# Attention in front of two MoE layers: how the softmax reciprocals reach the output rows, and a new order of the evictions

## What is computed

```python
q_rot, k_rot = rotate(q), rotate(k)                     # rotary embedding over D
scores = np.matmul(q_rot, k_rot.transpose(0, 1, 3, 2)) / np.sqrt(D)
attn = np.exp(scores - scores.max(-1, keepdims=True))
attn = attn / (attn.sum(-1, keepdims=True) + 1e-9)
x = np.matmul(attn, v)                                  # then heads side by side: 2304 x 512
gate, val = sigmoid(x @ w_gate), x @ w_val              # 512 -> 1536
x = (gate * val) @ w_out                                # 1536 -> 512
h = x @ w_in                                            # 512 -> 1024
ln = layernorm(h * softmax(h)) * g_ln
return ln @ w_out2                                      # 1024 -> 512
```

## Time and profile before

| | |
|---|---|
| median of the runs | 960.77 us (960.64 to 960.99) |
| profiled execution | 960.94 us, span 959.1 us |
| TensorE busy | 948.4 us (99%) |
| DVE busy | 508.2 us (53%) |
| ACT busy | 363.5 us (38%) |
| POOL busy | 339.1 us (35%) |
| attention | about the first 290 us of the span |

### The profile page before, as it was taken

One profiled execution on the slowest core, in us unless ns is written; L12 is line 12 of the kernel. 1 busy time (PEld: TensorE's weight loads), 2 busy tenths in 40 slices (PEclk: granted clock), 3 DMA queues, 4 the chain that ended last, 5 costly groups with the idle time before them and its releaser, 6 DMA issues.

```text
span 959.1 us, 15452 instructions
## 1 busy us (share of the span) xinstructions
PE 948.4 (99%) x5442; PEld 793.8 (83%) x5442; DVE 508.2 (53%) x890; ACT 363.5 (38%) x783; POOL 339.1 (35%) x246
## 2 busy tenths in 40 slices
PE   8999999999999999999999999999999999999998
PEld 6888888888876889888888888888888888888886
DVE  6898988989973343323234233243444554444441
ACT  5787787877862111111111111111111343333332
POOL 5556465564402904103202302401756432222200
PEclk9999999999999999999999999999999999999999
DMA  3333332333220120200100100100120011111111
GB/s 111 96 89 87 88 89 78 90 86 88 61 92 1 67 66 1 66 1 1 66 0 1 67 1 1 44 0 0 44 87 0 1 23 23 22 22 22 22 22 44
DMA packets 31842, 42.34 MB, mean 44 GB/s; under 512 B 5696, under 2 KB 20288, under 8 KB 31808
## 3 DMA queue, kind: packets, MB, share of 16 engines
q1 hardware_dynamic: 31664, 41.73, 15.6%
q10 hardware_dynamic: 144, 0.15, 0.1%
HBM read 28.30 MB, written 4.72 MB: 34 GB/s over the span
## 4 chain that ended last, share of the span: by engine, by line
PE 94%; ACT 1%; DVE 1%; issue 1%; POOL 1%; DMA 1%; SPq 0%; POOLq 0%; DVEq 0%
PE ps L1125 31%; PE ps L1169 15%; PE ps L1232 10%; PE ps L1062 9%; PE ps L1207 9%; PE ps L1107 8%; PE ps L1089 8%; PE ps L1029 2%; PE ps L1217 2%; PE ps L1000 1%; DMA raw_w<-in_moe_w_out 1%; DVE nmax L862 0%; ACT prob L702 0%; POOL x_lo L665 0%; POOL w_lo L554 0%
## 5 line engine op out<-in xcount | busy, mean ns | idle before, releaser
L1125 PE MATMUL ps<-x_hi,w_hi 128*128 128x512 f32 (+1 forms) x480 | 177.1, 369 | 0.2 <-POOL w_lo L554 0.2
L1125 PE MATMUL ps<-x_lo,w_hi 128*128 128x512 f32 (+1 forms) x480 | 176.7, 368 | 0.0
L1125 PE MATMUL ps<-x_hi,w_lo 128*128 128x512 f32 (+1 forms) x480 | 176.6, 368 | 0.0
L929 DVE TENSOR_TENSOR hid<-ps,sig 128x512 f32<-128x512 f32 (+1 forms) x60 | 38.3, 638 | 234.3 <-PE ps L1125 206.4
L741 ACT ACTIVATE sig<-ps 128x512 f32<-128x512 f32 (+1 forms) x60 | 33.3, 555 | 295.5 <-PE ps L1125 295.5
L1062 PE MATMUL ps<-kT,qT 128*128 128x288 f32 (+2 forms) x672 | 121.9, 309 | 2.3 <-ACT prob L702 1.9
L862 DVE TENSOR_REDUCE nmax<-ps 128x1 f32<-128x576 f32 x144 | 108.6, 755 | 23.3 <-PE ps L1062 19.4
L604 POOL TENSOR_SCALAR w_hi<-raw_w 128x1024 fp32r<-128x1024 f32 x15 | 41.3, 2778 | 210.5 <-PE ps L1169 210.5
L702 ACT ACTIVATE prob<-ps,nmax 128x576 f32<-128x576 f32 x128 | 94.2, 740 | 47.0 <-DVE nmax L862 45.7
L1125 PEld LDWEIGHTS ps<-x_hi,w_hi 128*128 128x128 f32 x480 | 90.5, 189 | 16.1 <-issue 0.9
L1125 PEld LDWEIGHTS ps<-x_hi,w_lo 128*128 128x128 f32 x480 | 90.5, 189 | 15.0
(11 more groups left out here) (120 smaller groups left out, 1659.2 us busy)
## 6 DMA issues: line engine op xcount, KB each, us to landing
kT<-kT SPq DMA_DIRECT2D x30, 288.0 KB, 3.7
raw_k<-in_k SPq DMA_DIRECT2D x16, 288.0 KB, 2.8
raw_q<-in_q SPq DMA_DIRECT2D x16, 288.0 KB, 3.1
out_y<-y_sb SPq DMA_DIRECT2D x36, 128.0 KB, 2.3
v_sb<-in_v SPq DMA_DIRECT2D x64, 64.0 KB, 2.3
raw_w<-in_moe_w_gate SPq DMA_DIRECT2D x6, 512.0 KB, 3.7
raw_w<-in_moe_w_val SPq DMA_DIRECT2D x6, 512.0 KB, 4.7
raw_w<-in_moe_w_out SPq DMA_DIRECT2D x6, 512.0 KB, 5.6
```

What stands on the lines that cost most here:

```text
L929: nc.vector.tensor_tensor(hid[:, f, 0:n], gv_ps[f][1][:, 0:n], sig[:, f, 0:n], ALU.mult).then_inc(hid_ready, 1)
L1125: last = nc.tensor.matmul(in_parts(gv_ps[f][n][:, 0:size(c)], c), w, x, start=m == 0, stop=m == len(todo) - 1)
```

## The change

1. INV writes its nine reciprocals to a block of 128 columns that is zero elsewhere. One transpose (RT) turns them, ACT copies nine rows of 128 to `rinv_t`, SP writes these to a DRAM tensor `inverses` (RW), waits, and reads them back to `rrep` by two DMAs whose source names each head's row 64 times (RR). `rwide`, R and KTR's third block are gone; KTR is now KT. `normal` waits for these DMAs (`rrep_in`). A slot order (`place`) puts the four rows of a head side by side.
2. kT and kTs hold the second head's last 64 keys a second time (one more piece of T), so that S8's products of the second head are two of 288 columns per part and no longer of 288, 224 and 64.
3. Evictions: ACT has A3, B1, TQ, B0, A0, B2, A1 and KT; DVE has A2, K and B3. Before, ACT had A0, B2, TQ, B0, A3, KTR and R, DVE A2, K, A1, B3 and B1.
4. New orders on all engines, SP's among them; POOL's RQ works one pair further ahead and XL one step earlier. SP issues the first weights in step 15 ahead of that step's RW.

```diff
-            kTT.append(alloc(at, f"kT{u}", [P, 4 * S + 2 * TAIL], F32R))
-            kT.append(kTT[u][:, 0:2 * S])
-            kTs.append(kTT[u][:, 2 * S:4 * S])
+            kTT.append(alloc(at, f"kT{u}", [P, 4 * S + 3 * TAIL], F32R))
+            kT.append(kTT[u][:, 0:2 * S + TAIL])
+            kTs.append(kTT[u][:, 2 * S + TAIL:4 * S + 2 * TAIL])
...
-        rinv = alloc(at, "rinv", [P, 2, SLOTS])
-        rwide = alloc(at, "rwide", [P, SLOTS, D])
+        rinv = alloc(at, "rinv", [P, 2, P])
+        rinv_t = alloc(at, "rinv_t", [SLOTS, P])
...
-        ORDER_PE = ["A2", "A0", "S0", "K", "B2", "S1", "A1", "B3", "S2", "TQ", "k", "S3", "T", "PV0", "KTR", "S4",
-                    "R", "q", "B1", "S5", "B0", "S6", "PV1", "S7", "A3", "S8"]
-
-        ORDER_ACT = ["A0", "S0", "B2", "S1", "TQ", "k", "T", "S2", "S3", "KTR", "R", "S4", "q", "B0", "S5", "S6",
-                     "S7", "A3", "S8"]
-
-        ORDER_DVE = ["A2", "S0", "K", "S1", "A1", "B3", "S2", "INV", "S3", "k", "T", "S4", "PV0", "S5", "S6", "q",
-                     "B1", "S7", "PV1", "S8"]
-
-        ORDER_POOL = ["RQ", "XL", "RK"]
-        FIRST_PE = ["S0", "S1", "S2", "k", "S3", "T", "S4", "S5", "q", "B1", "S6", "B0", "S7", "A3", "S8"]
-        FIRST_ACT = ["S0", "S1", "S2", "k", "S3", "T", "S4", "S5", "q", "S6", "B0", "S7", "A3", "S8"]
-        FIRST_DVE = ["S0", "S1", "S2", "S3", "k", "S4", "T", "S5", "S6", "q", "B1", "S7", "S8"]
-        AHEAD = {"A0": -1, "A1": -1, "A2": -1, "B2": -1, "B3": -1, "K": -1, "TQ": -1, "KTR": -1, "R": -1,
-                 "PV0": -1, "PV1": -1, "INV": -1, "XL": -2, "k": 1, "q": 1, "T": 1, "RQ": 1, "RK": 2}
+        ORDER_PE = ["A2", "S0", "A3", "K", "S1", "RT", "B1", "B3", "k", "S2", "KT", "T", "S3", "PV0", "S4", "TQ",
+                    "B0", "q", "S5", "A0", "S6", "PV1", "S7", "B2", "S8", "A1"]
+        ORDER_ACT = ["A3", "S0", "RT", "B1", "S1", "k", "S2", "T", "KT", "S3", "TQ", "S4", "B0", "q", "S5", "A0",
+                     "S6", "B2", "S7", "A1", "S8"]
+        ORDER_DVE = ["A2", "S0", "INV", "K", "S1", "B3", "S2", "S3", "k", "T", "S4", "PV0", "S5", "S6", "q", "S7",
+                     "PV1", "S8"]
+        ORDER_POOL = ["RK", "RQ", "XL"]
+        ORDER_SP = ["RW", "RR", "LK", "T", "LQ", "LV"]
+        FIRST_PE = ["S0", "S1", "S2", "k", "S3", "T", "S4", "B0", "S5", "q", "A0", "S6", "B2", "S7", "A1", "S8"]
+        FIRST_ACT = ["S0", "S1", "S2", "k", "S3", "T", "S4", "B0", "S5", "q", "A0", "S6", "B2", "S7", "A1", "S8"]
+        FIRST_DVE = ["S0", "S1", "S2", "S3", "k", "S4", "T", "S5", "S6", "q", "S7", "S8"]
+        AHEAD = {"A2": -1, "A3": -1, "B1": -1, "B3": -1, "K": -1, "TQ": -1, "KT": -1, "RT": -1, "PV0": -1, "PV1": -1,
+                 "INV": -1, "XL": -1, "k": 1, "q": 1, "T": 1, "RQ": 2, "RK": 2, "RW": -1, "RR": -1, "LK": 2, "LQ": 2,
+                 "LV": 1}
...
-                return [(around, q_tail, odd), (tails, k_tail, odd)]
+                again = keys[u][:, 2 * S:2 * S + TAIL]
+                return [(around, q_tail, odd), (tails, k_tail, odd), (again, k_tail[:, 1, :], odd)]
...
+        inverses = nc.dram_tensor("inverses", (SLOTS, P), F32, kind="Internal").ap()
+        def place(j):
+            return j % 2 * MT + j // 2 if j < 2 * MT else j
...
+            def write_inverses(p, step):
+                bank, before = use("RT", step)
+                sp.wait_ge(tr_out[bank], before + 1)
+                sp.dma_start(inverses, rinv_t[:]).then_inc(inverses_out, 16)
+            def spread_inverses(p):
+                sp.wait_ge(inverses_out, num(p) * 16 + 16)
+                main = inverses[0:2 * MT, :].rearrange("(h t) n -> h (t n)", h=2)
+                tails = inverses[2 * MT:SLOTS, :].rearrange("o (h n) -> (o h) n", h=2)
+                for src, a, b in ((main, 0, MAIN), (tails, MAIN, S)):
+                    sp.dma_start(rrep[:, a:b], src.unsqueeze(1).broadcast_to([2, D, b - a])).then_inc(rrep_in, 16)
             def step_in(name, p, step):
-                if name == "RK":
+                if step == PAIRS - 1 and name == "RW":
+                    for bank, before in newest(PIECES, PAIRS - 1):
+                        sp.wait_ge(tr_full[bank], before + 1)
+                    weights(0)
+                if name == "LK":
                     load(p, k, raw_k, k_in, k_prod)
-                elif name == "QN":
+                elif name == "LQ":
                     load(p, q, raw_q, q_in, q_prod)
                 elif name == "T":
                     swap(p, step)
-                elif name == "VN":
+                elif name == "LV":
                     load_v(p)
-
-            AHEAD.update(QN=2, VN=1)
+                elif name == "RW":
+                    write_inverses(p, step)
+                elif name == "RR":
+                    spread_inverses(p)
...
-                    held = ("K", "AB"[j % 2] + str(j // 2)) if j < 2 * MT else ("TQ", "KTR")
+                    held = ("K", "AB"[j % 2] + str(j // 2)) if j < 2 * MT else ("TQ", "KT")
...
-                                     accum_out=rsum[:, par(p), j, 0:1]).then_inc(exp_done, 1)
+                                     accum_out=rsum[:, par(p), place(j), 0:1]).then_inc(exp_done, 1)
...
-                if name in ("R", "KTR") and not early(p, 1):
-                    act.wait_ge(x_norm[1], num(p))
-                if name == "R":
-                    nc.scalar.activation(rrep[:, 0:MAIN], src, ACT.Copy).then_inc(tr_out[bank], 1)
+                if name == "RT":
+                    if not early(p, 1):
+                        act.wait_ge(x_norm[1], num(p))
+                    nc.scalar.activation(rinv_t[:], src[0:SLOTS, 0:P], ACT.Copy).then_inc(tr_out[bank], 1)
                     return
-                if name == "KTR":
-                    for h in range(2):
-                        r0 = h * TAIL
-                        nc.scalar.activation(rrep[r0:r0 + TAIL, MAIN:S],
-                                             src[r0:r0 + TAIL, 2 * P + r0:2 * P + r0 + TAIL], ACT.Copy)
                 for dst, part in p_parts(name, src, par(p)):
                     last = nc.scalar.activation(dst, part, ACT.Copy)
...
-                    bank, before = use("R", at_pair(p, -1 - AHEAD["R"]))
+                    bank, before = use("RT", at_pair(p, -1 - AHEAD["RT"]))
                     dve.wait_ge(tr_full[bank], before + 1)
                 u = par(p)
                 nc.vector.tensor_reduce(rtot[:, u, :], rsum[:, u, :, :], AX.X, ALU.add).then_inc(sum_eps, 1)
                 dve.wait_ge(sum_eps, num(p) + 1)
-                nc.vector.reciprocal(rinv[:, u, :], rtot[:, u, :]).then_inc(rinv_ready, 1)
-                dve.wait_ge(rinv_ready, num(p) + 1)
-                nc.vector.tensor_copy(rwide[:], rinv[:, u, :].unsqueeze(2).broadcast_to([P, SLOTS, D])
-                                      ).then_inc(wide_ready, 1)
+                nc.vector.reciprocal(rinv[:, u, 0:SLOTS], rtot[:, u, :]).then_inc(rinv_ready, 1)
             def normal(n, p, step):
                 a, b = SHARES[n]
-                bank, before = use("R", at_pair(p, -AHEAD["R"]))
                 dve.wait_ge(pv_done, num(p) * 2 + n + 1)
-                dve.wait_ge(tr_out[bank], before + 1)
+                dve.wait_ge(rrep_in, num(p) * 32 + 32)
                 if n == 0 and not early(p, 1):
                     dve.wait_ge(x_ready, num(p))
...
-                    todo[0] += [(zero_b, k_[:, b_main:b_main + half], 0) for k_ in both]
-                    todo[1] += [(zero_b, k_[:, b_main + half:], 0) for k_ in both]
-                    todo[1] += [(zero_b, k_[:, S:b_main], MAIN - half) for k_ in both]
+                    for b in range(2):
+                        todo[b] += [(zero_b, k_[:, b_main + b * half:b_main + (b + 1) * half], 0) for k_ in both]
...
-                if name == "KTR":
+                if name == "RT":
                     pe.wait_ge(rinv_ready, num(p) + 1)
-                if name == "R":
-                    pe.wait_ge(wide_ready, num(p) + 1)
                 if name == "K":
                     blocks = [prob[i][:, MAIN:MAIN + P] for i in range(MT)]
                 elif name == "TQ":
                     blocks = [prob_t[:, t * P:(t + 1) * P] for t in range(MT)]
-                elif name == "KTR":
-                    blocks = [prob_t[:, MAIN:MAIN + P], prob_t[:, MAIN - TAIL:S],
-                              rinv[:, par(p), 2 * MT:SLOTS].broadcast_to([P, P])]
-                elif name == "R":
-                    blocks = [rwide[:, 2 * i:2 * i + 2, :].rearrange("p h d -> p (h d)") for i in range(MT)]
+                elif name == "KT":
+                    blocks = [prob_t[:, MAIN:MAIN + P], prob_t[:, MAIN - TAIL:S]]
+                elif name == "RT":
+                    blocks = [rinv[:, par(p), :]]
...
-            BETWEEN = {"TQ": (0, 1), "PV0": (2,), "R": (3,)}
+            BETWEEN = {"KT": (0,), "TQ": (1, 2), "PV1": (3,)}
```

(56 more changed lines are left out.)

21 lines of the change are left out of this document (11 added, 10 removed).

## The result

The changed kernel takes 1043.11 us, median of 4 runs (1039.2 to 1046.88), beside 960.88 for the kernel before on the same chip: 1.0855 times as long, interval 1.0812 to 1.0899. The forecast was 991, with 1000 as its upper end. The sign was right and so was the mechanism (a narrow spread that TensorE waits for). The price was 52 us too low, because two further costs were missing: what the loads behind the spread do to it, and the clock that falls in the wait. The kernel before takes 960.79 to 961.02 beside the experiments, which ran on other chips, so times across them can be compared.

A forecast was written before the change was run, and what follows sets the result against it. TensorE was taken to bound the kernel. From 960.94 us, common terms gave -7.0 and the narrow spread 37.9 on top (14 x 2.2 plus 7.1), +30.9 in all: 991.8, stated as 991; range 952 to 1000.

The forecast's parts named there:

- What bounds the kernel: Attention pair of 17.16 us: TensorE busy throughout, clock full at 2.4 GHz; no part of the change turns on the clock.
- 0.24: Per pair, TensorE waits before RT (for the reciprocals) and B3 (for K's copy): 0.24 us together, bounds 0 and 0.5.
- The spread's time: Spread of inverses into rrep: two of 16 engines at 21.5 GB/s, tails landed at 12.5, PV1 2.2 us later per pair.
- rival b: SP's or DVE's order adds a second wait, such as swapped keys or raw_k behind the narrow spread: 1000; chance 0.08.
- The write: Write of 9 x 128 inverses to DRAM after RT's eviction: issued at 2.7, landed at 4.6 us of a step.
- What TensorE loses, and the new order: Per pair four transposes fewer (7.0 us in all), S8 0.17 shorter (2.7 in all); RT stands at 2.0, PV1 at 11.1.
- rival (a): The spread is as fast as the 288 KB load: 955.8, bounds 952.4 and 959.5, pair 16.85; chance 0.30.
- Step 15: Inverses' write queues behind the first weights; PV1 at 17.9: 7.1 us lost with a narrow spread, 1.9 with a fast one.
- Ends: Start: 0.6 us lost by ACT's extra pieces of T, 0.4 won in step 0; tail: 1.2 won.
- (c): Spread on more than two engines but not all, or short fixed part; landing past 10.1 costs 15 per us; chance 0.08.

The follow-up runs named there:

- e5_busy2: The changed kernel with 20 products of zeros ahead of PV1, so that TensorE isn't idle in the wait: 1026.42 us, 1.0682 of the kernel before.
- e1_wide: The changed kernel with the spread issued head by head, 64 target rows outermost, four transfers for two, same bytes: 957.75 us, 0.9961 of the kernel before.
- e10_both: The changed kernel with SP holding the following loads until the spread has landed, and 8 products of zeros ahead of PV1: 1002.86 us, 1.0446.
- e6_hold: The changed kernel with SP waiting until the spread has landed before issuing raw_k, the swap of keys and raw_q: 1004.83 us, 1.0457.
- e4_by4: The changed kernel with the spread as four transfers, each head's 64 rows written as 4x16 (4 entries outermost): 965.92 us, 1.0054.
- e2_by2: The changed kernel with the spread as four transfers, each head's 64 rows written as 2x32 (2 entries outermost): 1078.31 us, 1.1224.

## Why the prediction failed in size

**What bounds the kernel.** Right for the kernel before. The same paragraph said that no part of the change turns on the clock, and this is one of the two steps that failed. It was read off a kernel whose TensorE never waits in a steady pair; the forecast then put a wait of 2.2 us into each pair and kept the clock. The wait became 4.0, and PV1 to the next write took 10.34 for 8.6 at the full clock (e5_busy2): 1.74 a pair, 24 us. That the leg is 8.6 and not the 8.4 of the forecast is a sum of its own: PV1 was put 11.1 behind S0, but its terms (41 x 0.109, 7 x 0.53, 2.31, 0.1 and 0.24) come to 10.8, and e1_wide shows 10.9. That is 0.2 a pair, 3 us.

**The spread's time.** That two engines carry it was right (share 0.13; four, eight and 64 entries). Its size is the other step that failed: the leg was sized at 7.9 and took 10.13, 2.2 a pair, 31 us. Two terms of it were mis-sized. The first, some 21 us, is what the loads behind it add, a term that the forecast had at nothing: holding raw_k, the keys and raw_q back takes 1.5 off the leg. I saw that the keys and raw_k might land late behind the spread (rival b) and did not turn the question round: loads issued from 1.5 us behind the spread on make the spread late. The second, some 10 us, is the leg's own length, 8.4 to 8.6 with nothing behind it. The data moved faster than I took (25 GB/s an engine, not 21.5), but 288 KB at 50 GB/s are 5.9 us of the 8.4, so 2.5 lie outside them and not 1. I had taken 2 us as fixed for a load and then added only the half that I put before the first bytes. The spread of e10_both in slices of 0.5 us from 150.0 on, GB/s:

```profile
GB/s 33 2 7 0 0 16 41 57 49 49 49 53 53 49 49 49 35 36 3 0 0 46 207 310 328 214 185 335 246 185 235 217 149 38 124 106 47 12 33 0
```

It is issued at 151.45; its first bytes move shortly before 153, the last just behind 159.0, and x_f starts at 159.67: some 1.4 us stand ahead of the bytes and 0.6 behind them, and the last slices, with the tails, are slower than the rest (35 for 49).

**The write.** Landed in 1.24 us with SP's wake-up, where I took 1.9 from the small loads of the earlier trace rows: 0.66 a pair, 9 us won.

**The account.** -9.2 (write) + 31.2 (spread) + 1.5 (x_f to PV1, 0.11 a pair) + 24.4 (clock) + 2.8 (the rest of PV1 to the next write) = 50.7 of the 52.1 us between 991 and 1043.1, and of 53.8 to the profiled execution; step 15 and the ends are not in it. The same table gives the three experiments: 14 times the difference of a pair from the changed kernel's is 16 us for e5_busy2 (measured 16.7 between the medians, 18.7 between the profiled executions), 38 for e6_hold (38.3 and 39.4), 42 for e10_both (40.2 and 42.9). The terms are not independent: the loads lengthen the wait and the wait lowers the clock, so that holding the loads alone gives 38 us back, 21 of them in the spread's leg.

**What TensorE loses, and the new order.** Right. e1_wide is rival (a), forecast at 955.8 with 952.4 to 959.5, measured 957.75. Its pair is 16.84 us (S0 of step 1 at 29.11, of step 15 at 264.93) for 16.85; RT stands 2.03 after S0 (149.73, 147.70) for 2.0. Of the 0.24 that I gave to waits at RT and B3 at most 0.1 shows, at RT (S1 to RT takes 0.61 here and 0.70 in the next pair); where the rest of it lies I did not find. The rows of a steady pair of e1_wide:

```profile
147.70 0.79 PE L1082 MATMUL ps<-kT,qT 128*128 128x288 f32 x4
149.12 0.78 PE L1082 MATMUL ps<-kT,qT 128*128 128x288 f32 x4
149.73 0.28 PE L1106 MATMUL ps<-eye_f,rinv 128*128 128x128 f32 x1
...
158.60 2.37 PE L1124 MATMUL ps<-pT,v_sb 128*64 128x320 f32 x16
```

PV1 stands 10.9 after S0 (forecast 11.1) and nothing precedes it but products.

**Step 15.** PV1 stood 18.6 after S0 in the changed kernel (345.71, 364.31) for a forecast of 17.9, so the queue behind the weights was sized well. What I missed is the clock again: even with the wide spread PV1 there takes 4.53, and the step takes 4.7 us more than in the kernel before (5.0 if the shorter pair is counted apart, as in the forecast), where I had 1.9. Moving the weights gave 2.2 of them back (955.59).

**Ends.** In e1_wide the wait of S0 for ACT's copy is 0.68 for 0.31 and S0 starts at 14.08 for 13.85: 0.2 lost, not 0.6. From the first transposes of step 16 to the end it wins 1.4 us on the kernel before, for the 1.2 of the forecast.

**Rivals and chances.** (b) had a mechanism near the true one with the wrong direction: raw_k and the keys did land late, but TensorE waits for neither in the changed kernel. (c) was excluded by the share of 0.13; its slack was right (e4_by4, whose x_f comes 6.2 after the issue, has TensorE wait for it in 8 pairs, 6.6 us in all). The range ended at 1000 because it was made of the bounds of the landing time alone, with the speed of TensorE fixed.

## What to carry to other kernels

Where a change puts a wait into a loop in which TensorE never waited, price the work behind the wait at both levels of the clock, and write the loop as a ring of legs: once something waits in each turn, every leg counts in full, and the ring shows which ones have been forgotten. Broadcast over partitions with the target's rows as the outermost entries of the transfer and one source row per transfer, not with a source of two rows. And when a transfer is on few engines, look at what is issued right behind it, since it is both delayed and a cause of delay; eight entries would have been enough here.

## What the runs showed of the hardware

- A transfer from DRAM to SBUF whose outermost count is 2 ran at a DMA share of 0.13 and 50 GB/s, with 4 at 0.23, 8 at 0.36 (0.48 in 1 us of it) and 64 at 0.60. Cut into twice as many transfers, the form with 2 moved 31 GB/s at the same 0.13 (e2_by2), which stays open. The Trainium skill, DMA: Bandwidth & Descriptors, "Rules for kernel authors", says that a transfer uses no more engines than its slowest dimension has entries: these runs agree.
- Loads of 288 and 304 KB with 64 or 128 rows outermost that were issued behind such a transfer landed after 10.1 us in place of 2.8 (raw_k) and 8.7 in place of 3.7 (keys), and the transfer itself came to use 1.5 us later for them.
- A write of 4.5 KB to DRAM and the wake-up of the queue that waits for it took 1.24 us.
- After 3.73 us of idle time TensorE ran at half pace (16 matmuls in 4.54 us for 2.37) for the whole of PV1; after 3.64 us, seven pairs on, it kept its full pace. After 1.90 us it kept it in one place (e6_hold) and not after 2.29 in another pair of that run, nor after 1.88 in e1_wide (step 15, where 0.91 us of idle stood shortly before). So the length of one gap alone doesn't decide. Products of zeros in the gap kept the clock at 1.00.
